# A 64-step linear-attention scan feeding two feed-forward layers on one core: the first stage's levels taken block by block in two PSUM regions, weight splitting moved to VectorE and spread into the second stage, the last u_lo put ahead of x_lo, and half the keys in level five

## The reference, cut to what matters

```python
for t in range(S):                       # attention: B=4, H=8, S=768, D=48
    cur = einsum('bhd,bhe->bhde', u[None] * kt, vt)
    y[:, :, t] = einsum('bhd,bhde->bhe', rt, state + cur)
    state = wt[:, :, :, None] * state + einsum('bhd,bhe->bhde', kt, vt)
# gated layer, 3072 tokens, 384 -> 1536 -> 384
xn = x / sqrt(mean(x * x) + 1e-6) * rms_g
x1 = (silu(xn @ w_gate) * (xn @ w_val)) @ w_out
# squared layer, 384 -> 2048 -> 384
out = (s * relu(x1 @ w_in) ** 2 + b) @ w_out2
```

## Time and profile before

| | |
|---|---|
| device time, 3 runs | median 1092.07 us (1091.19 to 1098.44) |
| the profiled execution | 1089.28 us, its span 1087.1 us |
| granted TensorE clock, mean | 0.989 |
| PE busy | 1045.3 us, 96% of the span |
| DVE, ACT, POOL busy | 516.9, 339.8, 269.8 us |

### The profile page before, as it was taken

How to read it: one execution, slowest core, us unless ns; L and a number is a source line. 1 busy time by engine, 2 the same in 40 slices (tenths; PEclk the granted TensorE clock), 3 DMA queues, 4 the chain that set the end, 5 groups by cost and what they waited for, 6 DMA issues and landing times. The chain is left out here.

```text
span 1087.1 us, 26414 instructions
## 1 busy us (share of the span) xinstructions
PE 1045.3 (96%) x11492; PEld 905.3 (83%) x11492; DVE 516.9 (48%) x662; ACT 339.8 (31%) x607; POOL 269.8 (25%) x193
## 2 busy tenths in 40 slices
PE   5788999999999999999999999999999999999998
PEld 5787888788788878887888788789898998989988
DVE  4976742773376437634753222580614417053250
ACT  3143133223322341223132333551614326052240
POOL 3894520462055216502540023230000000000000
PEclk9899999999999999999999999999999999999999
DMA  8450032003101311040000400321001010010000
GB/s 303 177 157 22 31 108 69 31 32 126 51 33 59 114 54 42 31 147 30 32 2 3 172 3 1 100 82 51 1 22 36 7 51 0 22 36 14 15 0 29
DMA packets 21986, 62.37 MB, mean 57 GB/s; under 512 B 2816, under 2 KB 6272, under 8 KB 21888
## 3 DMA queue, kind: packets, MB, share of 16 engines
q1 hardware_dynamic: 21456, 60.24, 16.2%
q10 hardware_dynamic: 432, 0.67, 0.2%
HBM read 51.46 MB, written 9.44 MB: 56 GB/s over the span
## 5 line engine op out<-in xcount | busy, mean ns | idle before, releaser
L1132 DVE SCALAR_TENSOR_TENSOR sqr<-relu,sb_col 128x512 f32<-128x512 f32 x96 | 80.5, 840 | 207.6 <-ACT relu L1083 206.1
L844 POOL TENSOR_TENSOR R<-R,arena 128x512 f32<-128x512 f32 x72 | 116.1, 1631 | 197.8 <-PE level_ps L338 173.1
L774 DVE TENSOR_TENSOR u_raw<-value_ps,u_raw 128x512 f32<-128x512 f32 x72 | 49.8, 692 | 198.2 <-PE value_ps L464 198.0
L609 ACT ACTIVATE u_raw<-gate_ps 128x512 f32<-128x512 f32 x72 | 43.1, 598 | 221.2 <-PE gate_ps L464 221.2
L476 PE MATMUL o_ps<-u_hi,wo_hi 128*128 128x512 f32 x216 | 90.3, 418 | 12.4 <-DVE u_lo L778 12.3
L701 DVE TENSOR_TENSOR K<-K,arena 128x512 f32<-128x512 f32 x72 | 84.2, 1180 | 32.4 <-PE level_ps L338 31.9
L338 PEld LDWEIGHTS level_ps<-R,K 64*64 64x64 f32 x4608 | 76.1, 143 | 25.1 <-issue 18.8
L1051 PE MATMUL o_ps<-wt_hi,g_lo 128*128 128x384 f32 x288 | 96.2, 334 | 0.0
L1051 PE MATMUL o_ps<-wt_lo,g_hi 128*128 128x384 f32 x288 | 96.2, 334 | 0.0
L1051 PE MATMUL o_ps<-wt_hi,g_hi 128*128 128x384 f32 x288 | 96.2, 334 | 0.0
L615 ACT ACTIVATE u_hi<-u_raw 128x512 fp32r<-128x512 f32 x72 | 45.5, 632 | 158.9 <-DVE u_raw L774 158.9
(11 more groups left out here) (120 smaller groups left out, 2144.3 us busy)
## 6 DMA issues: line engine op xcount, KB each, us to landing
kr_nat<-kr SPq DMA_DIRECT2D x12, 768.0 KB, 4.4
K<-kT SPq DMA_DIRECT2D x12, 512.0 KB, 3.6
arena<-wT SPq DMA_DIRECT2D x12, 512.0 KB, 4.4
R<-rT SPq DMA_DIRECT2D x11, 512.0 KB, 3.7
v_sb<-v SPq DMA_DIRECT2D x12, 384.0 KB, 4.3
w_raw<-wgv SPq DMA_DIRECT2D x12, 384.0 KB, 12.9
x_scratch<-x_sb SPq DMA_DIRECT2D x18, 256.0 KB, 3.2
x_raw<-x_scratch SPq DMA_DIRECT2D x6, 768.0 KB, 4.5
```

The costliest lines, as they stand in the source:

```text
L609: act.activation(u[:, f % 2], gate_ps[:], ACT.Silu).then_inc(silu_done, 1)
L774: dve.tensor_tensor(u[:, f % 2], value_ps[:], u[:, f % 2], ALU.mult).then_inc(u_done, 1)
L844: pool.tensor_tensor(q, q, decay(blk, l, 0), ALU.mult).then_inc(rmul_done, 1)
L1132: dve.scalar_tensor_tensor(out=sq[f % 2][:], in0=relu[f % 2][:], scalar=sb_col[:, 0:1], in1=relu[f % 2][:], op0=ALU.mult, op1=ALU.mult).th ...
```

## The change

1. Levels of stage 0 go block by block: `level(s, l, blk)`, with `place` of one block at a time, and block 1 of stage 0 writes to two banks of its own (`o01_ps`, which are the output banks of the gated layer, unused in stage 0). VectorE does keys, place for block 0, keys, place for block 1, and then the next level's decays. Level 0 of both blocks starts as the data lands; `keep_busy(24)` becomes `keep_busy(8)`, with `keep_busy(3)` after each block's level. SP loads decays ahead of the second keys; ScalarE's queue loads both queries.
2. GpSimd lowers no w or wo any more. VectorE lowers w 0, 1, 2 and wo 0 in step 18 of stage 0, w 3, wo 1 and w 4 in steps 24 and 26, and the other seven w and four wo pieces in stage 1. ScalarE makes w_hi in steps 0 to 11 and wo_hi in steps 12 to 14, which is ahead of `place_near`.
3. `sum_alpha` of block 0 goes from step 6 to 9, of block 1 from step 15 to 18; GpSimd's `own_keys` and `own_products` move with them.
4. attend of block 1 goes from step 25 to 26, the third and fourth state update from step 23 to 24, `turn_x` becomes one group of 12 transposes in step 29 (NEXT_AT = 34, TURN_AT = 29), packed in three banks, and `x_out` one group of 12.
5. In step 34 VectorE lowers u (f = 11) and only then x; level 0 of the next stage, its decays, keys and queries go to step 34 too, between output 10 and output 11; its `place` goes to step 1 of the next stage.
6. Level 5 loads 32 keys as weights instead of 64.

```diff
-BUSY = {3: 12, 6: 12, 9: 12, 12: 12, 15: 10, 18: 6, 20: 6, 22: 3, 23: 6, 24: 3, 25: 16, 28: 8, 30: 8}
+TURN_AT, NEXT_AT = 29, 34
+LATE_WEIGHTS = (8, 11, 14, 17, 20, 23, 25)
+LATE_OUT = (7, 16, 21, 27)
+BUSY = {15: 4, 18: 12, 20: 6, 22: 3, 24: 3, 26: 20, 29: 12}
...
+            keys = HALF if l == NEAR else SUB
+            for q in range(Q):
+                for i in range(2):
+                    for h in range(2):
+                        rows = slice(h * SUB, (h + 1) * SUB)
+                        first_key = q * P + i * SUB
+                        mm = pe.matmul(pairs_ps(s, blk)[i * SUB:i * SUB + keys, h * Q + q, blk * HALF:(blk + 1) * HALF],
+                                       K[blk][rows, first_key:first_key + keys],
+                                       halves(R[blk][rows, first_key:first_key + SUB], l)[:, :, 1],
+                                       start=True, stop=True, skip_group_check=True)
...
 # TensorE
             if k in LEVEL_AT:
-                level(s, LEVEL_AT.index(k) + 1)
+                for blk in range(2):
+                    level(s, LEVEL_AT.index(k) + 1, blk)
+                    if s == 0:
+                        keep_busy(3)
...
+            if k == NEXT_AT and s + 1 < NSB:
+                for blk in range(2):
+                    level(s + 1, 0, blk)
...
 # ScalarE
-            if s == 0 and 3 <= k < 3 + F1:
-                upper_weights(k - 3)
+            if s == 0 and k < F1:
+                upper_weights(k)
+            if s == 0 and k in (12, 13, 14):
+                for j in range(2):
+                    upper_out_weights(2 * (k - 12) + j)
             if k == LEVEL_AT[-1]:
                 place_near(s)
-            if s == 0 and k in (16, 17):
-                for j in range(3):
-                    upper_out_weights(3 * (k - 16) + j)
             if k == TOP_AT:
                 place_far(s)
...
 # VectorE
+        def keys_after(s, l):
+            for blk in range(2):
+                multiply_keys(s, l, blk)
+                if s == 0 and l < NEAR:
+                    place(s, l, blk, 1)
...
-            if k == LEVEL_AT[1]:
-                sum_alpha(2 * s)
-            if k == LEVEL_AT[4]:
+            if k == LEVEL_AT[2]:
+                sum_alpha(2 * s)
+            if k == TOP_AT:
                 if s == 0:
+                    lower_weights(0)
+                    lower_weights(1)
                 sum_alpha(2 * s + 1)
+                if s == 0:
+                    lower_weights(2)
+                    lower_out_weights(0)
...
+            if s == 1 and k in LATE_WEIGHTS:
+                lower_weights(5 + LATE_WEIGHTS.index(k))
+            if s == 1 and k in LATE_OUT:
+                lower_out_weights(2 + LATE_OUT.index(k))
-            if k == 33:
+            if k == NEXT_AT:
                 lower_x(s)
+                if s + 1 < NSB:
+                    decays_after(s + 1, 0)
+                    keys_after(s + 1, 0)
...
 # GpSimd
-                if s == 0:
-                    lower_weights(2 * l - 2)
...
-            if s == 0 and k in (19, 20, 21, 22, 23, 24):
-                lower_out_weights(k - 19)
+            if k == NEXT_AT and s + 1 < NSB:
+                multiply_queries(s + 1, 0)
```

More of the change, by code:

```diff
@@ L98, in level_no, with placed, copied, attention_and_gated_phase @@
     return 2 * (LV * s + l) + blk + 1
-def attention_and_gated_phase(nc, a, whole, first, x1_dram, x1_out, x_hi, x_lo, level_ps, mix_ps, gate_ps, value_ps, o_ps):
+def placed(s, l, blk):
+    return 2 * l + blk + 1 if s == 0 else NEAR * (s + 1) + l + 1
+def copied(s, blk):
+    return 2 * (blk + 1) if s == 0 else 2 * (s + 2)
+def attention_and_gated_phase(nc, a, whole, first, x1_dram, x1_out, x_hi, x_lo, level_ps, mix_ps, gate_ps, value_ps, o01_ps, o_ps):
     def sem(name):
@@ L325, in _, with level @@
     def _(pe):
-        def level(s, l):
-            level_out(pe, s, l - 1)
+        def level(s, l, blk):
+            level_out(pe, s, l - 1, blk)
             if l == 0 and s > 0:
                 wait(pe, xe_done, KT * CH * s)
[L330 to L341, removed]
@@ L343, in top_level @@
-        def top_level(s):
-            l = LV - 1
[L346 to L357, removed]
+            keys_ready(pe, s, l, blk)
@@ new lines, in level, with top_level @@
+            mm.then_inc(level_done, 1)
+        def top_level(s, blk):
+            l = LV - 1
+            level_out(pe, s, l - 1, blk)
+            keys_ready(pe, s, l, blk)
+            queries_ready(pe, s, l, blk)
+            for p in range(NP):
+                for c in range(C):
+                    for h in range(2):
+                        rows, q = slice(h * SUB, (h + 1) * SUB), c * NP + p
+                        mm = pe.matmul(pairs_ps(s, blk)[c * SUB:(c + 1) * SUB, h * Q + blk * NP + p],
+                                       K[blk][rows, q * P:q * P + SUB], R[blk][rows, q * P + SUB:(q + 1) * P],
+                                       start=True, stop=True, skip_group_check=True)
+            mm.then_inc(level_done, 1)
@@ L444, in attend, with turn_x @@
                     mm.then_inc(y_done, 1)
[L446 to L454, removed]
+        def turn_x(s):
+            wait(pe, norm_done, CH * (s + 1))
+            for n in range(CH):
+                y = y_sb[n][:].rearrange("p (i k) -> p k i", k=KT)
+                for k in range(KT):
+                    mm = pe.transpose(xt_ps[n][k], y[:, k], eye[:])
             mm.then_inc(xt_done, 1)
@@ L1172, in build @@
         bank = {name: whole.enter_context(nc.psum_tensor(name, [P, 512], F32))
[L1173 to L1174 removed]
+                for name in ("mix_ps", "gate_ps", "value_ps", "o_ps2")}
+        o01_ps = whole.enter_context(nc.psum_tensor("o01_ps", [P, 2 * 512], F32))
+        o_ps = [o01_ps[:, 0:512], o01_ps[:, 512:1024], bank["o_ps2"][:]]
         win_hi, win_lo = attention_and_gated_phase(nc, a, whole, first, x1_dram, x1_out, x_hi, x_lo, level_ps,
[L1176 removed]
+                                                   bank["mix_ps"], bank["gate_ps"], bank["value_ps"], o01_ps, o_ps)
         first.close()
```

233 lines of the change are left out of this document (124 added, 109 removed).

## The result

| | before | after |
|---|---|---|
| device time, 4 runs each | 1092.30 us (1091.19 to 1098.44) | 1065.55 us (1063.83 to 1066.80) |
| the profiled execution, its span | 1089.28, 1087.1 | 1065.07, 1063.3 |
| granted TensorE clock, mean | 0.989 | 0.986 |

What follows compares the result with a forecast made beforehand. TensorE, busy 96% of the span, was taken as the bound, leaving its gaps, its own work and stage 0. Gains 21.7 + 2.2 + 2.3 - 0.5 = 25.7 off 1092.07 gave 1066.4 us, range 1056 to 1075.

Steps and rivals of the forecast that it cites:

- gate 0 at 84 to 90: Sign of being right: the first gate matmul of stage 1 starts 84 to 90 us into the execution.
- no o_ps wait for u_lo: Sign of being right: at stage ends TensorE's output 11 no longer waits for u_lo, before five times 2.46 us.
- `place_near` directly behind wo_hi: Sign in stage 0: ScalarE's near copy follows wo_hi, released by or right after the wo DMA; TensorE idles some 10 us.
- u ahead of x and level 0 moved: Stage ends: output 10 and level 0 cover u_lo; gaps of 12.3 and 3.0 and low clock go, 21.7 us gained.
- Half the keys: Level 5, stages 1 to 5: 32 weight columns gain 4.7 us if columns alone limit, else 0; middle 2.3 taken.
- rival C: Half the keys in level 5 give nothing, another floor at 14.6 ns: 1068.7 us; chance 0.35 within the forecast.
- Stage 0, +2.2: Stage 0: levels finish earlier, late wo loads hold level 6; gate 0 at 87.0 to 87.5, gain 2.2 us.
- From 20.0 that makes 35.0: Stage 0, levels 1 to 3 at VectorE's 6.4, 4.7 and 3.9 us: done at 35.0, alpha of block 0 at 36.0.
- Moved pieces: VectorE's 11 more weight pieces in stage 1 and later alpha of block 1: 0.5 us charged (0 to 3).
- Rival B: VectorE's queue becomes a new bound in stages 1 to 5, giving back 5 to 15: 1072 to 1081 us; chance 0.12.
- D: Slower than before: VectorE's queue at its worst, 40 us lost against 25.7, 1106 us; chance 0.02.
- Rival A: Stage 0: wo loads don't hold level 6 back; gate 0 near 79, gain 10, 1058 us; chance 0.13.

Runs made afterwards that it cites:

- run 5: The kernel before with only VectorE's x_lo moved behind u_lo of f = 11 (step 34 instead of 33): 1074.16 us, ratio 0.9863.
- run 6: The changed kernel with x_lo back in step 33, ahead of u_lo, level 0 left between outputs 10 and 11: 1080.24 us, ratio 0.9898.
- run 4: The changed kernel with 64 keys as weights in level 5 again: 1067.67 us, ratio 0.9734.
- Run 3: The changed kernel without keep_busy(3) behind each block's level in stage 0: 1066.61 us, ratio 0.9731.
- runs 1 and 2: Changed kernel with wo loads issued ahead of block 1's k and r, 1059.74 us; changed kernel with wo_hi behind the last keys_out, wo_lo 0 later, 1057.67 us.
- run 11: The changed kernel once more, unedited: 1065.98 us, ratio 0.9759.
- run 7: The changed kernel with keep_busy(6) instead of keep_busy(3) behind each block's level of stage 0: 1068.34 us, ratio 0.9774.
- run 9: The changed kernel with wo loads ahead, stage 0's VectorE weight pieces and block 1's alpha behind the state operations, and keep_busy(6) in the levels: 1059.01 us.

## Why the prediction came out as it did

The time, 1066.4 against 1065.55, came out right, in part by luck: stages 1 to 6 gave 26.7 where 23.5 were forecast, stage 0 had the wrong sign, and the median before happened to lie high (see the result). Of the signs named in the prediction, gate 0 at 84 to 90 failed (92.44), and stage 0's -3.0 lies outside its own bounds of -2 to +6. The others held: no o_ps wait for u_lo, PEclk at 1.00 from 64 on, `place_near` directly behind wo_hi, level 5 at 1.35 us.

*u ahead of x and level 0 moved, 21.7: right.* The traces give 12.3 + 3.05 of gaps and, by run 5, 5.3 of clock: 20.7. (The sums in the prediction should read 21.3 and 22.1; 21.7 is their middle.) Runs 5 and 6 test the order from both sides: alone it gains 17.6, undone it costs 12.7. The cover that I named for x_lo held (189.72 against 191.94). What I didn't see is that the moved level 0, without the reordering, still leaves a gap of 1.76 in four stages.

*Half the keys, 2.3: the mechanism right, the size off.* Measured 3.5 (run 4), 0.7 a stage. The bound by weight columns alone was 0.93 a stage. By rows, the start to start of two of these matmuls is (1.35 - 0.22)/127 = 8.9 ns with 32 weight columns, 14.6 with 64. So cost does go mostly by weight columns, and rival C is out. The Trainium skill's section on the back-to-back issue gap ("TensorE: Matmul & The Clock Gate") puts starts at least some 25 ns apart; the measurement is a third of it for these tiles.

*Stage 0, +2.2: wrong, it was -3.0.* The step that failed is the one that walks through the levels by VectorE's work alone ("From 20.0 that makes 35.0"). TensorE's added fill ran at the low clock and made a level 6.9 us; alpha ended at 39.6, not 36.0. Run 3, without that fill, put it at 35.9; run 4, with the fill at the high clock, at 37.4. Both the fill and the clock it ran at were left out of the walk. The next steps were right and passed the error on: the last wo 16.0 behind alpha (15.8), `place_near` directly behind wo_hi, level 6 3.65 late. The tail from level 6 to gate 0 added 1.5: I had 33.4 us for it and it took 34.9. 0.5 of it is there at the state (12.6 us instead of 12.1). Behind level 6 alpha of block 1 waits 1.71 us for GpSimd's product. VectorE's two slow w pieces (4.28 instead of my 3.0) are done by then, though GpSimd's rows beside them are slow too (2.52 and 2.42 where the same rows of block 0 took 1.89 and 1.81). The 12 fill products at the low clock (4.93) delay the updates, but these end at 68.9, and VectorE reaches the state copy only at 70.15, straight behind wo_lo. The other 1.0 lies between state and gate 0: the "issue" gap of 1.7 in the second attend, less what was forecast too long. Nor would the levels as forecast have brought stage 0's gain: run 3 has them, and its gate 0 is at 92.02.

*Moved pieces, -0.5: nothing.* No matmul of stages 1 to 5 waits for VectorE in the wait list. Rival B and D didn't happen; the slack that I counted at step 18 was enough.

*What is left over* is some 2.5 us in stages 1 to 5 that no term had: 26.7 less 12.3, 3.05, 5.3 and 3.5, which is also what lies between run 5 and the changed kernel (9.1) less 3.05 and 3.5. Fewer switches of TensorE between groups may be it (`turn_x` in one group, level 0 between two outputs instead of ahead of gate 0). No run took these apart.

*Rival A* was no outcome of this change, but runs 1 and 2 show it as an edit: with the hold lifted stage 0 gives 5.8 to 7.5 us. Gate 0 came at 86.67 and 84.97 there, not at its 79. Whether the levels at VectorE's pace would add the rest is open: no run put loads ahead and no fill together.

*Still open:* what sets where the clock falls within stage 0. The changed kernel repeats its pattern in its second profile (run 11), but run 4, the same program up to level 5, doesn't. In both trials with double fill (7, 9) alpha came 1.1 to 1.5 us earlier and gate 0 2.3 to 3.0 later.

## What to carry to other kernels

Where a filler is there to keep TensorE's clock up, count it as work in the chain at the lower clock, and ask which engine then sets the pace; here a filler of 1.65 us per block cost 3.7 us at alpha. Then follow the gain to the end of the stage: taking that filler away gave the 3.7 back at alpha and nothing at gate 0. Before you put work earlier in an engine's queue, ask what it depends on: wo_hi waited for a load, the load for a VectorE result, and `place_near`, which needed neither, waited for both. Two moves into one place must be costed together: u_lo beside GpSimd's product takes 1.98 us, ahead of it 0.69.

## What the runs showed of the hardware

- *The clock can be low without a gap.* From 28 to 47 TensorE is busy 19.00 of 19.00 us, and the granted clock is 0.50, i.e. 1.2 GHz, in levels of 64x64 tiles and unit products; before it fell TensorE had stood still 1.8 us. In run 4 it stood still 1.9 us at the same place in the same program, and the clock stayed at 1.00 until 49.5. With double fill (run 7) the stretch was at 1.00 with 17.88 busy. What decides is not shown.
- *TensorE stops without a wait that the profile shows while the DMA engines are all busy.* After, 1.7 us in the second attend:

```profile
74.80:78.80 4.00, 2.28 (x70) 1.98 (x67) 2.02 (x4) 1.12 (x4) 0.89 (x2) 1.00 1.02 400
```

  The DMA share is 1.02 there, 1.01 in run 9's stretch. Packets of the DMA queue that the page calls "instruction" landed 1.4 us before each of the two longest such gaps of the changed kernel ended. That late instructions are the cause is argued from this and not shown: no run moved the loads of stage 1 alone.
- *A VectorE row can take nearly three times as long beside GpSimd:* u_lo, 128x512, 1.98 us at the four stage ends of run 6 where a GpSimd product started just before it, 0.69 at the fifth. None of the 35 u_lo rows of that run without a GpSimd product beside them takes over 0.70.
